# Query features of the later pairs transposed by VectorE and DMA moves instead of TensorE

## The chip, the cores and the metric

The kernel runs on one core of a Trainium2 chip. The metric is the device time of one execution in microseconds; lower is better. TensorE (PE) multiplies, VectorE (DVE), ScalarE (ACT) and GpSimd (POOL) work element by element, SyncE (SP) issues most transfers; ScalarE can issue transfers too.

## The reference

Attention with random features, and behind it two gated feed-forward layers:

```
q, k, v: (4 batches, 8 heads, 576 tokens, 64), omega: (128, 64)
phi(x) = exp(h - max(h)) / sqrt(128),  h = x @ omega.T - |x|^2 / 2   (x scaled)
kv = phi(k).T @ v,  z = sum over tokens of phi(k)
attention = phi(q) @ kv / (phi(q) @ z + 1e-6)
x = attention as (2304 tokens, 512)
h = x @ w_in (512 x 2048);  x = (h * clip(h + 3, 0, 6) / 6) @ w_out (2048 x 512)
h = x @ w_in2;              out = (h * sigmoid(1.702 h)) @ w_out2
```

## The kernel before, in words

Heads are worked on in 16 pairs `a`, four a batch. Pairs 0 to 4 come ahead of the feed-forward layers; pairs 5 to 15 (`a >= LEAD`) are woven into the first layer. Each layer works on five chunks of tokens (four of 512, one of 256) and 16 blocks of 128 inner features (J = 16) a chunk, so step `n` is one block of one chunk: `hidden(n)` makes it (12 matmuls), ScalarE's `gate(n)` and VectorE's `gated_block(n)` gate it, ScalarE's `high(n)` and VectorE's `low(n)` part it in two numbers that add up to it, `output(n)` multiplies it (12 matmuls). Every product is made of three: high by high, low by high, high by low. `hidden(n)` waits for `gated_block(n-1)`, as both use one PSUM bank; `output(n)` waits for `low(n)`. TensorE's order is hidden(n), the units of slot 2n, output(n-1), the units of slot 2n+1.

A pair takes eight slots, `UNITS`. With n0 = 2 + 4(a - 5), slot 0 lies behind output(n0-1), slot 2 (k) behind output(n0), slot 5 (kv) behind hidden(n0+3). The units are: the projections of q with the tails, and of k; the two turns; the key-value sums; two halves of the numerator. After a projection VectorE takes maxima and biases (`statistics`), ScalarE the exponentials (`exps`, tiles of 128 tokens by 128 features). 576 tokens are four tiles and a tail of 64; the tails of two heads share a tile. The numerator needs q's features by feature, not by token: `turn` (L553) transposes four tiles of a head on TensorE, `key_values` (L561) the tail tile; ScalarE copies the turned bank as the high part (L762) and VectorE subtracts it for the low part (L985). `keep` (L972 to L980) parts the sums and the turned tails. The numerator (L614 to L616) makes numerator and denominator at once; `quotient_part` copies them, `normalise` divides.

SP's queue is an order written out by hand: in slot 2 the next pair's key rows, in slot 3 its columns, in slot 6 query rows and values, and in every even slot the weights of step n+5 (until step 15). POOL squares the rows for the norms and makes the weights' low parts, ScalarE the weights' high parts three steps ahead. At the first step of a chunk (`n % J == 0`) both engines evacuate the former chunk's sums; at the last step of a chunk ScalarE (L811) and VectorE (L1063) split the next chunk's input.

Of the kernel before, what the change touches and what calls it, by code (L numbers as in the profile page):

```python
# [11 lines left out]
P = 128  # L12
D = 64
# [9 lines left out]
UNITS = (("q", "tail"), (), ("k",), ("turn0",), ("turn1",), ("kv",), ("nd0",), ("nd1",))  # L23
# [4 lines left out]
def build(nc, q_t, k_t, q_n, k_n, v_n, v_tail, omega_t, w_in, w_out, w_in2, w_out2, out):  # L28
# [24 lines left out]
    with ctx:  # L53
# [32 lines left out]
        q_lo = sb("q_lo", [P, 2, S], F32R)  # L86
# [4 lines left out]
        q_hi = nc.alloc_sbuf_tensor_at("q_hi", [P, 2, S], F32R, offset=(phi_base + 31) // 32 * 32)  # L91
# [32 lines left out]
        turned_out = sem("turned_out")  # L124
        q_lo_ready = sem("q_lo_ready")
# [142 lines left out]
        def tile_of(a, kind, h, t):  # L268

            if t == ST:  # L270
                return (q_tail_b if in_set_b(a) else q_tail_a)[:] if kind == KQ else phi_of(a, kind)[:, 2 * ST * FEAT:GROUPS * FEAT]
            return phi_of(a, kind)[:, (h * ST + t) * FEAT:(h * ST + t + 1) * FEAT]
# [58 lines left out]

        block = ctx.enter_context(nc.Block())

        @block.sync
        def _(sp):
# [40 lines left out]

            sp.dma_start(omega2[0:D, :], omega_t).then_inc(load_omega, 16)
# [121 lines left out]
        def _(pe):  # L499
# [42 lines left out]
            def turn(a, h):  # L542
                pe.wait_ge(exp_done, banks_to(a, "q", h))
                if 0 < a < LEAD - 1 and h == 0:
                    pe.wait_ge(tails_out, a)
                    if a > 1:
                        pe.wait_ge(x_written, 2 * (a - 1))
                elif a < LEAD - 1 and h == 1:
                    pe.wait_ge(turned_out, 2 * a + 1)
                elif a >= LEAD:  # L550
                    pe.wait_ge(exp_done, banks_to(a, "tail", 0) if h == 0 else banks_to(a, "k", 0))
# [4 lines left out]
            def key_values(a):  # L556
# [4 lines left out]
                nc.tensor.transpose(bank[:, 0:P], tile_of(a, KQ, 0, ST), ident[:])  # L561
# [34 lines left out]
            def numerator(a, half):  # L596
                pe.wait_ge(state_ready, a + 1)
                if half == 0:
                    pe.wait_ge(turned_out, 2 * a + 2)
                    if a == LEAD - 1:  # L600
                        pe.wait_ge(gated, 2)
                else:
                    pe.wait_ge(tails_out, a + 1)
                    if a == LEAD - 1:
                        pe.wait_ge(x_written, 2 * a)
# [12 lines left out]
            def attend(a, what):  # L618
                if what in ("q", "k", "tail"):
                    projection(a, what)  # L620
                elif what in ("turn0", "turn1"):
                    turn(a, int(what == "turn1"))
                elif what == "kv":
                    key_values(a)
                else:
# [107 lines left out]
        def _(act):  # L733
# [29 lines left out]

            def first_high(a):
# [16 lines left out]
            def attend(a, what):  # L781
                if what in ("q", "tail", "k"):
                    exps_of(a, what)
                elif what in ("turn0", "turn1"):
                    turned_head(a, int(what == "turn1"))
# [89 lines left out]
            for n in range(2 * L2):  # L875
                former, now = slot_units(2 * n - 1), slot_units(2 * n)
                for a, what in former:
                    if what in ("q", "k"):
                        exps(a, what, 0)
                    elif what != "tail":  # L880
                        attend(a, what)
                gate(n)
                for a, what in former:
                    if what in ("q", "k"):
                        exps(a, what, 1)
                for a, what in now:
# [17 lines left out]
                for a, what in now:  # L904
                    if what not in ("nd0", "nd1"):
# [11 lines left out]
        def _(dve):  # L917
# [40 lines left out]
            def keep(a):  # L958
# [11 lines left out]
                den, num = sums[:, :, D:D + 1].to_broadcast([P, 2, D]), sums[:, :, 0:D]  # L970
                tails, q = bank[:, 0:P].rearrange("p (h s) -> p h s", h=2), q_hi[:, :, ST * P:S]
                nc.vector.tensor_copy(state_hi[:, 1:3, :], den).then_inc(high_set, 1)  # L972
                nc.vector.tensor_copy(state_hi[:, 0:4:3, :], num).then_inc(high_set, 1)
                nc.vector.tensor_copy(q, tails).then_inc(high_set, 1)
                dve.wait_ge(high_set, 3 * (a - LEAD + 1) + 1)
                nc.vector.tensor_tensor(state_lo[:, 1:3, :], den, state_hi[:, 1:3, :].bitcast(F32), ALU.subtract)
                dve.wait_ge(high_set, 3 * (a - LEAD + 1) + 2)
                nc.vector.tensor_tensor(state_lo[:, 0:4:3, :], num, state_hi[:, 0:4:3, :].bitcast(F32), ALU.subtract).then_inc(state_ready, 1)
                dve.wait_ge(high_set, 3 * (a - LEAD + 1) + 3)
                nc.vector.tensor_tensor(q_lo[:, :, ST * P:S], tails, q.bitcast(F32), ALU.subtract).then_inc(tails_out, 1)  # L980
# [67 lines left out]
            def attend(a, what):  # L1048
# [6 lines left out]
                elif what in ("turn0", "turn1"):  # L1055
                    turned_low(a, int(what == "turn1"))
# [80 lines left out]
            for n in range(2 * L2):  # L1137
                before, former, now = (slot_units(2 * n - i) for i in (2, 1, 0))
                for a, what in former:
# [4 lines left out]
                    elif what in ("kv", "turn0", "turn1"):  # L1144
# [4 lines left out]
                gated_block(n)  # L1149
# [5 lines left out]
                for a, what in now:  # L1155
                    if what == "nd0":
                        normalise(a, 0)
                    else:
                        attend(a, what)
                low(n)  # L1160
                if n == 0:
# [65 lines left out]
```

## Time and profile before

| | us |
|---|---|
| median of 3 runs | 930.99 (930.59 to 931.5) |
| the profiled execution, its own time | 932.24 |
| its span, first to last instruction | 930.4 |
| TensorE busy | 923.9 (99%) |
| VectorE busy | 419.3 (45%) |
| ScalarE busy | 378.8 (41%) |
| GpSimd busy | 170.6 (18%) |

Durations of matmuls overlap, since they are pipelined; what one costs is read from the starts. The granted TensorE clock is at full speed in every slice.

### The profile page before, as it was taken

What the parts mean: (1) busy time and instruction counts of PE and PEld (TensorE: products, weight loads), DVE (VectorE), ACT (ScalarE), POOL (GpSimd) and SP (SyncE); (2) the same over time, 40 slices, a digit from 0 to 9 for tenths busy, and PEclk for the clock granted to TensorE, in tenths of its full rate; (3) what the DMA queues carried; (4) which work ended last, traced back from release to release, by engine and by line L of the source; (5) the groups of instructions that cost most, each with busy time, mean ns of one, the idle gap of its engine ahead of it and who ended that gap; (6) DMA issues with size and microseconds to landing.
All of it is one profiled execution on the core that took longest, in us unless ns stands there. A gap on an engine that the chain in (4) does not pass through costs nothing.

```text
span 930.4 us, 13097 instructions
## 1 busy us (share of the span) xinstructions
PE 923.9 (99%) x5130; PEld 785.9 (84%) x5130; DVE 419.3 (45%) x801; ACT 378.8 (41%) x869; POOL 170.6 (18%) x182
## 2 busy tenths in 40 slices
PE   8999999999999999999999999999999999999998
PEld 8988888888888888888889988888888888888898
DVE  6966667655656566532233532242224222422322
ACT  6856565445445454432235732232223222322322
POOL 1765654212122110000007820000000000000000
PEclk9999999999999999999999999999999999999999
DMA  8644341221212210000004600010001000100000
GB/s 273 188 118 132 98 133 27 64 64 39 55 36 64 55 35 14 13 33 1 1 1 137 181 1 1 1 46 1 1 0 46 1 1 0 46 1 1 16 31 24
DMA packets 44254, 46.01 MB, mean 49 GB/s; under 512 B 25120, under 2 KB 25760, under 8 KB 44192
## 3 DMA queue, kind: packets, MB, share of 16 engines
q1 hardware_dynamic: 43680, 44.42, 16.3%
q8 instruction: 41, 0.67, 0.3%
q10 hardware_dynamic: 512, 0.75, 0.3%
q14 instruction: 21, 0.17, 0.1%
HBM read 40.44 MB, written 4.72 MB: 49 GB/s over the span
## 4 chain that ended last, share of the span: by engine, by line
PE 96%; DVE 1%; POOL 1%; DMA 1%; ACT 1%; issue 0%; ACTq 0%; DVEq 0%; POOLq 0%
PE acc L682 14%; PE acc L684 14%; PE acc L683 14%; PE hid L656 11%; PE hid L632 10%; PE hid L657 10%; PE att L657 4%; PE att L656 4%; PE att L632 4%; PE att L569 3%; PE att L531 3%; PE att L553 1%; PE acc L531 1%; PE att L517 1%; PE att L614 1%; PE att L616 1%
## 5 line engine op out<-in xcount | busy, mean ns | idle before, releaser
L682 PE MATMUL acc<-g_hi,w_out_hi 128*128 128x512 f32 (+1 forms) x640 | 237.7, 371 | 0.1
L684 PE MATMUL acc<-g_hi,w_out_lo 128*128 128x512 f32 (+1 forms) x640 | 235.9, 369 | 0.0
L683 PE MATMUL acc<-g_lo,w_out_hi 128*128 128x512 f32 (+1 forms) x640 | 235.6, 368 | 0.0
L656 PE MATMUL hid<-x_hi,w_in_hi 128*128 128x512 f32 (+1 forms) x476 | 179.2, 376 | 0.9 <-DVE R L1071 0.8
L657 PE MATMUL hid<-x_hi,w_in_lo 128*128 128x512 f32 (+1 forms) x476 | 175.2, 368 | 0.0
L632 PE MATMUL hid<-x_lo,w_in_hi 128*128 128x512 f32 (+1 forms) x476 | 175.2, 369 | 0.0
L1078 DVE TENSOR_TENSOR g_lo<-R,g_hi 128x512 fp32r<-128x512 f32 (+1 forms) x160 | 107.9, 674 | 82.8 <-ACT g_hi L828 82.6
L684 PEld LDWEIGHTS acc<-g_hi,w_out_lo 128*128 128x128 f32 x640 | 120.6, 188 | 20.4
L682 PEld LDWEIGHTS acc<-g_hi,w_out_hi 128*128 128x128 f32 x640 | 120.8, 189 | 19.4 <-issue 0.5
L683 PEld LDWEIGHTS acc<-g_lo,w_out_hi 128*128 128x128 f32 x640 | 120.8, 189 | 18.9
L828 ACT ACTIVATE g_hi<-R 128x512 fp32r<-128x512 f32 (+1 forms) x160 | 94.8, 592 | 84.6 <-DVE R L1073 52.6
L656 PEld LDWEIGHTS hid<-x_hi,w_in_hi 128*128 128x128 f32 x476 | 89.7, 189 | 16.4 <-DVE R L1071 1.6
L632 PEld LDWEIGHTS hid<-x_lo,w_in_hi 128*128 128x128 f32 x476 | 89.8, 189 | 15.5 <-DVE x_lo L1038 0.2
L657 PEld LDWEIGHTS hid<-x_hi,w_in_lo 128*128 128x128 f32 x476 | 89.9, 189 | 13.6
L1071 DVE SCALAR_TENSOR_TENSOR R<-R,hid 128x512 f32<-128x512 f32 (+1 forms) x79 | 49.8, 631 | 107.7 <-ACT R L819 107.7
L819 ACT ACTIVATE R<-hid 128x512 f32<-128x512 f32 (+1 forms) x79 | 43.9, 556 | 105.1 <-PE hid L632 105.1
L1073 DVE TENSOR_TENSOR R<-R,hid 128x512 f32<-128x512 f32 (+1 forms) x40 | 25.4, 634 | 112.9 <-ACT R L821 112.9
L1073 DVE TENSOR_TENSOR R<-R,att 128x512 f32<-128x512 f32 (+1 forms) x40 | 25.4, 634 | 112.8 <-ACT R L821 112.8
L821 ACT ACTIVATE R<-att 128x512 f32<-128x512 f32 (+1 forms) x40 | 22.2, 555 | 116.8 <-PE att L632 116.2
L821 ACT ACTIVATE R<-hid 128x512 f32<-128x512 f32 (+1 forms) x40 | 22.2, 555 | 115.9 <-PE hid L632 115.9
L1044 DVE RECIPROCAL k_phi<-k_phi 128x288 f32<-128x288 f32 x24 | 46.8, 1949 | 31.6 <-ACT k_phi L774 31.6
L657 PE MATMUL att<-x_hi,w_in_lo 128*128 128x512 f32 (+1 forms) x164 | 60.4, 368 | 0.0
(165 smaller groups left out, 1096.8 us busy)
## 6 DMA issues: line engine op xcount, KB each, us to landing
X<-w_in SPq DMA_DIRECT2D x16, 256.0 KB, 2.6
X<-w_out SPq DMA_DIRECT2D x16, 256.0 KB, 2.9
out_t<-X SPq DMA_DIRECT2D x16, 256.0 KB, 2.2
rows<-q_n SPq DMA_DIRECT2D x13, 288.0 KB, 3.2
rows<-k_n SPq DMA_DIRECT2D x13, 288.0 KB, 3.0
v_rows<-v_n SPq DMA_DIRECT2D x14, 256.0 KB, 3.3
q_cols<-q_t SPq DMA_DIRECT2D x11, 256.0 KB, 2.5
k_cols<-k_t SPq DMA_DIRECT2D x11, 256.0 KB, 2.7
```

What stands on the lines that cost most here:

```text
L632: return nc.tensor.matmul(hid_bank(n)[:, 0:t], w_hi[0][:, s * 512 + k * P:s * 512 + (k + 1) * P], x_lo[:, k, x0:x0 + t], start=False, stop ...
L656: nc.tensor.matmul(bank, w_hi[0][:, at], x_hi[:, k, x0:x0 + t], start=(k == 0), stop=False)
L657: nc.tensor.matmul(bank, w_lo[0][:, at], x_hi[:, k, x0:x0 + t], start=False, stop=False)
L682: nc.tensor.matmul(bank, w_hi[1][:, at], g_hi[:, g, 0:t], start=(s == 0), stop=False)
L683: nc.tensor.matmul(bank, w_hi[1][:, at], g_lo[:, g, 0:t], start=False, stop=False)
L684: last = nc.tensor.matmul(bank, w_lo[1][:, at], g_hi[:, g, 0:t], start=False, stop=(s == J - 1))
L821: nc.scalar.activation(R[:, 0:t], h, ACT.Sigmoid, scale=1.702).then_inc(gate_ready, 1)
L828: nc.scalar.activation(g_hi[:, n % G_SLOTS, 0:t], R[:, 0:t], ACT.Copy).then_inc(g_hi_ready, 1)
L1044: nc.vector.reciprocal(d, d).then_inc(recip_done, 1)
L1071: nc.vector.scalar_tensor_tensor(out=r, in0=r, scalar=6.0, in1=h, op0=ALU.min, op1=ALU.mult).then_inc(gated, 1)
L1073: nc.vector.tensor_tensor(r, r, h, ALU.mult).then_inc(gated, 1)
L1078: nc.vector.tensor_tensor(g_lo[:, n % G_SLOTS, 0:t], R[:, 0:t], g_hi[:, n % G_SLOTS, 0:t].bitcast(F32), ALU.subtract).then_inc(g_ready, 1)
```

## The change

For pairs 5 to 15 TensorE transposes nothing more. Host code rotates the tokens of the second head by 64 in these pairs (`in_order`), and q's tiles are laid out as head 0, the shared tail, head 1. VectorE transposes the 32x32 blocks of the whole q buffer in two instructions (`cross`, 512 and 640 columns) into `q_blocks`. Then sixteen DMAs (`block_move`), each of 32 partitions by 9 groups by 32 elements, put the blocks in their places in the q buffer: SP issues the twelve off the diagonal, ScalarE the four on it. ScalarE copies each head's 576 columns as the high part (`parts0`, `parts1`), VectorE subtracts for the low part. `keep` no longer handles tails.

The order around it changes too. SP issues the next pair's key rows in slot 1, then waits for `cross` and issues its twelve moves, ahead of the columns and the weights. ScalarE's four moves come at the end of step n0+2, the parts at step n0+3. At the first step of a chunk VectorE's gated product stands ahead of the key statistics, and ScalarE's gate and high part ahead of the key exponentials.

```diff
-UNITS = (("q", "tail"), (), ("k",), ("turn0",), ("turn1",), ("kv",), ("nd0",), ("nd1",))
+UNITS = (("q", "tail"), ("cross",), ("k",), ("moves",), (), ("parts0", "kv", "parts1"), ("nd0",), ("nd1",))
...
-        q_lo = sb("q_lo", [P, 2, S], F32R)
+        blocks_base = nc.sbuf_base
+        q_blocks = sb("q_blocks", [P, 2 * S])
...
+        def block_move(i, j):
+            to = phi_a[KQ][j * 32:(j + 1) * 32, :].rearrange("p (g c) -> p g c", g=GROUPS)
+            blocks = q_blocks[i * 32:(i + 1) * 32, :].rearrange("p (g c) -> p g c", g=GROUPS)
+            return to[:, :, i * 32:(i + 1) * 32], blocks[:, :, j * 32:(j + 1) * 32]
...
+            def moves(a):
+                sp.wait_ge(crossed, 2 * (a - LEAD) + 2)
+                for i in range(4):
+                    for j in range(4):
+                        if j != i:
+                            sp.dma_start(*block_move(i, j)).then_inc(moved[i], 16)
...
             for g in range(2 * LAST1):
-                a = at_slot(g, 2)
+                a = at_slot(g, 1)
                 if a is not None and LEAD <= a < PAIRS - 1:
                     rows_of(a + 1, KK)
+                if a is not None and LEAD <= a:
+                    moves(a)
                 a = at_slot(g, 3)
...
-                nc.tensor.transpose(bank[:, 0:P], tile_of(a, KQ, 0, ST), ident[:])
+                if a < LEAD:
+                    nc.tensor.transpose(bank[:, 0:P], tile_of(a, KQ, 0, ST), ident[:])
...
+            def moves(a):
+                act.wait_ge(crossed, 2 * (a - LEAD) + 2)
+                for i in range(4):
+                    nc.scalar.dma_start(*block_move(i, i)).then_inc(moved[i], 16)
+
+            def high_features(a, h):
+                for i in range(4):
+                    act.wait_ge(moved[i], 64 * (a - LEAD + 1))
+                nc.scalar.activation(q_hi[:, h, :], phi_a[KQ][:, h * S:(h + 1) * S], ACT.Copy).then_inc(turned_out, 1)
...
-                former, now = slot_units(2 * n - 1), slot_units(2 * n)
+                former, now, first = slot_units(2 * n - 1), slot_units(2 * n), n % J == 0
                 for a, what in former:
                     if what in ("q", "k"):
-                        exps(a, what, 0)
+                        if not first:
+                            exps(a, what, 0)
...
                 gate(n)
+                if first:
+                    high(n)
                 for a, what in former:
                     if what in ("q", "k"):
+                        if first:
+                            exps(a, what, 0)
                         exps(a, what, 1)
                 for a, what in now:
-                    if what in ("nd0", "nd1"):
+                    if what in ("nd0", "nd1", "parts0"):
                         attend(a, what)
                 if n % J == J - 1 and n < 2 * L2 - 1:
                     next_chunk(n)
-                high(n)
+                if not first:
+                    high(n)
...
-                if n % J == 0 and n > 0:
+                if first and n > 0:
                     evacuate(n // J - 1)
+                for a, what in now:
+                    if what == "moves":
+                        moves(a)
...
+            def cross(a):
+                split_at = ST * FEAT
+                dve.wait_ge(exp_done, banks_to(a, "q", 0))
+                nc.vector.transpose(q_blocks[:, 0:split_at], phi_a[KQ][:, 0:split_at]).then_inc(crossed, 1)
+                dve.wait_ge(exp_done, banks_to(a, "tail", 0))
+                nc.vector.transpose(q_blocks[:, split_at:2 * S], phi_a[KQ][:, split_at:2 * S]).then_inc(crossed, 1)
+
+            def low_features(a, h):
+                dve.wait_ge(turned_out, 2 * a + h + 1)
+                nc.vector.tensor_tensor(q_lo[:, h, :], phi_a[KQ][:, h * S:(h + 1) * S], q_hi[:, h, :].bitcast(F32),
+                                        ALU.subtract).then_inc(q_lo_ready, 1)
...
+                if n % J == 0:
+                    gated_block(n)
                 for a, what in former:
                     if what in ("q", "k"):
                         attend(a, what)
...
-                gated_block(n)
+                if n % J > 0:
+                    gated_block(n)
...
                 low(n)
+                for a, what in now:
+                    if what == "cross":
+                        attend(a, what)
```

## Rows read from the trace of the kernel before

**Rows 1.** The waits of TensorE, the longest: total us, times, longest.
```profile
PE att L540 <- DVE state L1091: 1.1, 1, 1.1
```

**Rows 2.** Timeline of TensorE, first transposes of pairs 6 and 10.
```profile
105.25 0.60 PE L553 MATMUL att<-ident,q_phi 128*128 128x128 f32 x4
...
224.00 0.60 PE L553 MATMUL att<-ident,q_phi 128*128 128x128 f32 x4
```

**Rows 3.** Instructions of line L553: duration ns min/median/max, first and last start us.
```profile
L553 PE MATMUL att<-ident,q_phi x104: 270/272/328, 9.8 to 375.9; 128*128 128x128 f32 x104
```

**Rows 4.** Timeline of TensorE in pair 10: start us, duration us, instruction.
```profile
223.77 0.39 PE L632 MATMUL hid<-x_lo,w_in_hi 128*128 128x512 f32 x1
...
224.67 0.39 PE L683 MATMUL acc<-g_lo,w_out_hi 128*128 128x512 f32 x1
...
226.97 0.39 PE L684 MATMUL acc<-g_hi,w_out_lo 128*128 128x512 f32 x1
...
227.87 0.39 PE L657 MATMUL hid<-x_hi,w_in_lo 128*128 128x512 f32 x1
...
230.18 0.39 PE L632 MATMUL hid<-x_lo,w_in_hi 128*128 128x512 f32 x1
...
230.74 1.90 PE L569 MATMUL att<-v_rows,k_phi 128*128 128x65 f32 x16
...
235.31 0.29 PE L614 MATMUL att<-q_hi,state_hi 128*128 128x288 f32 x1
```

**Rows 5.** Timeline of VectorE in pair 10.
```profile
219.61 0.69 DVE L1078 TENSOR_TENSOR g_lo<-R,g_hi 128x512 fp32r<-128x512 f32 x1
...
221.25 1.29 DVE L933 TENSOR_REDUCE row_max<-att 128x4 f32<-128x512 f32 x2 [0.74 <-PE att L531]
...
222.85 0.17 DVE L951 SCALAR_TENSOR_TENSOR bias<-h_max,half_norm 128x8 f32<-128x8 f32 x1
224.83 0.69 DVE L1071 SCALAR_TENSOR_TENSOR R<-R,hid 128x512 f32<-128x512 f32 x1 [1.80 <-ACT R L819]
...
232.68 0.29 DVE L972 CAST state_hi<-att 128x128 fp32r<-128x128 f32 x1 [0.75 <-PE att L569]
```

**Rows 6.** The page's groups of instructions: count, busy us, mean ns, idle before.
```profile
L1044 DVE RECIPROCAL k_phi<-k_phi 128x288 f32<-128x288 f32 x24 | 46.8, 1949 | 31.6 <-ACT k_phi L774 31.6
```

**Rows 7.** Timeline of ScalarE in pair 10.
```profile
223.06 1.14 ACT L756 ACTIVATE k_phi<-att,bias 128x128 f32<-128x128 f32 x4 [2.83 <-DVE bias L951]
224.20 0.60 ACT L819 ACTIVATE R<-hid 128x512 f32<-128x512 f32 x1
```

**Rows 8.** Transfers of lines L358, L346 (column tails), L427 (stores): ns, landing us.
```profile
L358 SPq DMA_DIRECT2D rows<-k_n x13: 333/429/1314, 10.4 to 323.9; - x13
...
L346 SPq DMA_DIRECT2D q_cols<-q_t x11: 596/597/597, 48.9 to 340.9; - x11
...
DMA to landing us min/median/max: 2.1/2.2/3.7
...
DMA to landing us min/median/max: 1.7/2.0/2.5
```

**Rows 9.** Windows: stretch, busy us of engines, clock, DMA share, GB/s.
```profile
353.00:354.00 1.00, 1.00 (x6) 0.83 (x5) 0.50 (x2) 0.00 (x0) 0.00 (x0) 1.00 0.99 226
```

**Rows 10.** Timeline of VectorE in pair 6.
```profile
103.90 0.35 DVE L948 SCALAR_TENSOR_TENSOR h_max<-row_max,half_norm 128x8 f32<-128x8 f32 x1
104.29 1.21 DVE L951 SCALAR_TENSOR_TENSOR bias<-h_max,half_norm 128x8 f32<-128x8 f32 x1
```

**Rows 11.** Timeline of GpSimd in pair 6.
```profile
104.19 1.29 POOL L458 TENSOR_TENSOR w_out_lo<-X,w_out_hi 128x512 fp32r<-128x512 f32 x1
109.19 1.15 POOL L447 TENSOR_TENSOR rows<-rows 128x576 f32<-128x576 f32 x1 [3.71 <-DMA rows<-k_n]
```

**Rows 12.** Timeline of TensorE in pair 8, behind hidden(16).
```profile
164.48 0.60 PE L553 MATMUL att<-ident,q_phi 128*128 128x128 f32 x4
```

**Rows 13.** Timeline of VectorE in pair 8, the low part of step 15.
```profile
163.31 0.69 DVE L1078 TENSOR_TENSOR g_lo<-R,g_hi 128x512 fp32r<-128x512 f32 x1
```

**Rows 14.** Timeline of ScalarE in pair 8, the evacuation.
```profile
169.40 1.16 ACT L834 ACTIVATE X<-acc 128x512 f32<-128x512 f32 x2
```

More of the change, by code:

```diff
@@ L124, in build @@
         turned_out = sem("turned_out")
+        crossed = sem("crossed")
+        moved = [sem(f"moved{i}") for i in range(4)]
         q_lo_ready = sem("q_lo_ready")
@@ L268, in tile_of @@
         def tile_of(a, kind, h, t):
+            if kind == KQ and a >= LEAD:
+                g = ST if t == ST else h * (ST + 1) + t
+                return phi_of(a, KQ)[:, g * FEAT:(g + 1) * FEAT]
             if t == ST:
@@ L599, in numerator @@
                     pe.wait_ge(turned_out, 2 * a + 2)
-                    if a == LEAD - 1:
+                if a == LEAD - 1:
+                    if half == 0:
                         pe.wait_ge(gated, 2)
-                else:
-                    pe.wait_ge(tails_out, a + 1)
-                    if a == LEAD - 1:
+                    else:
+                        pe.wait_ge(tails_out, a + 1)
                         pe.wait_ge(x_written, 2 * a)
@@ L783, in attend @@
                     exps_of(a, what)
-                elif what in ("turn0", "turn1"):
-                    turned_head(a, int(what == "turn1"))
+                elif what in ("parts0", "parts1"):
+                    high_features(a, int(what == "parts1"))
                 elif what in ("nd0", "nd1"):
@@ L969, in keep @@
                     return
-                den, num = sums[:, :, D:D + 1].to_broadcast([P, 2, D]), sums[:, :, 0:D]
-                tails, q = bank[:, 0:P].rearrange("p (h s) -> p h s", h=2), q_hi[:, :, ST * P:S]
+                den, num, made = sums[:, :, D:D + 1].to_broadcast([P, 2, D]), sums[:, :, 0:D], highs_to(a - 1)
                 nc.vector.tensor_copy(state_hi[:, 1:3, :], den).then_inc(high_set, 1)
                 nc.vector.tensor_copy(state_hi[:, 0:4:3, :], num).then_inc(high_set, 1)
-                nc.vector.tensor_copy(q, tails).then_inc(high_set, 1)
@@ L980, in keep @@
-                nc.vector.tensor_tensor(q_lo[:, :, ST * P:S], tails, q.bitcast(F32), ALU.subtract).then_inc(tails_out, 1)
+                if a < LEAD:
+                    tails, q = bank[:, 0:P].rearrange("p (h s) -> p h s", h=2), q_hi[:, :, ST * P:S]
+                    nc.vector.tensor_copy(q, tails).then_inc(high_set, 1)
+                    dve.wait_ge(high_set, made + 3)
+                    nc.vector.tensor_tensor(q_lo[:, :, ST * P:S], tails, q.bitcast(F32), ALU.subtract).then_inc(tails_out, 1)
@@ L1054, in attend @@
                         take_tails(a - 1)
-                elif what in ("turn0", "turn1"):
-                    turned_low(a, int(what == "turn1"))
+                elif what == "cross":
+                    cross(a)
+                elif what in ("parts0", "parts1"):
+                    low_features(a, int(what == "parts1"))
             def split(c, blocks_k=range(KC), part=None):
@@ L1143, in _ @@
                         normalise(a, 0)
-                    elif what in ("kv", "turn0", "turn1"):
+                    elif what == "kv":
                         attend(a, what)
@@ L1157, in _ @@
                         normalise(a, 0)
-                    else:
+                    elif what != "cross":
                         attend(a, what)
                 low(n)
+                for a, what in now:
+                    if what == "cross":
+                        attend(a, what)
                 if n == 0:
@@ L1187, with in_order @@
     pairs, full = B * H // 2, S // P
+    def in_order(x):
+        y = x.reshape(pairs, 2, S, Dh).copy()
+        y[LEAD:, 1] = np.roll(y[LEAD:, 1], full * P - S, axis=1)
+        return y
     def cols(x):
-        return np.ascontiguousarray(x.transpose(0, 1, 3, 2).reshape(pairs, 2 * Dh, S))
+        return np.ascontiguousarray(in_order(x).transpose(0, 1, 3, 2).reshape(pairs, 2 * Dh, S))
     def tiles(x):
-        y = x.reshape(pairs, 2, S, Dh)
+        y = in_order(x)
         return y[:, :, :full * P].reshape(pairs, 2, full, P, Dh), y[:, :, full * P:]
```

18 lines of the change are left out of this document (8 added, 10 removed).

## The prediction

> **What bounds the kernel.** In the table above TensorE is busy all through, VectorE and ScalarE less than half. I then read TensorE's waits: none is over 1.1 us [rows 1]. So the end moves by work taken off TensorE or by waits put onto it. The timelines of one pair, at 212 to 240 us (pair 10), show how near each helper is to its due time. Pair 6's first transposes start at 105.25, pair 10's at 224.00: 29.7 us a pair [rows 2]. Every time below is read, or shifted, in such a timeline.
>
> **Taken off TensorE.** L553 transposes eight tiles a pair, L561 one; eleven pairs (5 to 15) lose them, 88 of the first kind among these [rows 3]. Matmuls of 512 columns start 0.23 us apart: ten intervals from 224.67 to 226.97 [rows 4]. Over the first four transposes, from 223.77 to the second matmul behind them at 224.67, it is 0.90 where two starts take 0.46: 0.44 us. Over the second four 0.90 again: 0.44. Over the tail's 0.56 less 0.46: 0.10. Sum 0.98 a pair, times 11 = **10.8 us**, all of it on the engine that bounds. The copies and subtractions that read turned PSUM banks become ones of 576 SBUF columns, about 0.7 us as now.
>
> **Added to VectorE: two 32x32 transposes, 512 and 640 columns, behind the low part of step n0+1.** No row shows this operation. Nearest: the two-input subtraction of 512 columns, 0.69 us, the next start after 0.6; at the near end a maximum, 1.29 for two of 512 [rows 5]; far off the reciprocal, 1.95 for 288 columns, so 7.8 us for 1152 [rows 6]. I take the subtraction's rate, since this too is a plain stream: 0.6 + 0.8 = 1.4 us. Behind them stand the norms (0.2) and the key maxima: 219.61 + 0.6 + 1.4 + 0.2 = 221.8 for 221.25, some 0.6 late. Late next: key exponentials at 223.7 for 223.06, gate at 224.8 [rows 7], gated product ended at 226.1 (now 224.83 + 0.69). Hidden block n0+3 waits for that product and now comes at 226.97 - 0.44 + 0.23 = 226.76. Covered, 0.6 to spare.
>
> **Added to the queues: sixteen moves of 36 KB, 288 pieces of 128 B each.** SP issues twelve once the blocks are ready (221.7). Issues took 0.33 to 1.31 us on SP; the half-width column tails, which the moves resemble most, landed 2.2 after issue, 3.7 at the longest, stores out of SBUF at 1.7 at the least [rows 8]. I take 0.6 with the gap for an issue (between the median 0.43 and the long ones) and 2.3 for landing. SP's last move starts at 221.7 + 11 x 0.6 = 228.3, landed 230.6. The transfer engines' own time: values are 1152 pieces of 256 B a pair, drained around 353 to 355 in some 1.4 us of all sixteen, 0.99 of it in one us [rows 9]; that is 20 ns a piece on one engine. At that price the moves take 288 x 20 ns = 5.8 us of each engine, inside the issue time. ScalarE issues its four after the high part of n0+2: exponentials 223.7, gate 224.8, second half 225.3, high 226.2 to 226.9; last issue 228.7, landed 231.0. Queued behind its issues (2.4 us, to 229.3) is gate(n0+3), whose hidden block ends at 230.18 + 0.23 - 0.88 = 229.5: in time. Behind SP's twelve (7.2 us) wait the next pair's columns, query rows and values: the columns land near 235, and two more blocks of TensorE follow the numerator (235.31) before they are read. Nobody waits.
>
> **The parts.** ScalarE: head 0 from 231.0 to 231.7, high(n0+3) to 232.3, head 1 to 232.9. VectorE: low of head 0 to 232.5, the state's four operations 0.2 apart (as from 232.68, [rows 5]) to 233.3, low of head 1 to 234.0. The numerator's first head is due at 235.31 - 0.98 = 234.3, its second at 234.7 [rows 4]. Covered, by 0.7. So the ordinary pairs (9, 10, 11, 13, 14, 15) keep their 0.98, but a landing more than 0.7 later is paid for one to one.
>
> **Pairs 5 to 7**, where POOL still splits weights. Pair 6's bias, a small operation of two SBUF inputs, took 1.21 us and ended with POOL's subtraction at 105.5; in pair 10 the same is 0.17 [rows 5, 10, 11]. Now the first of the two small operations (103.90) comes 1.35 later, at 105.25, still behind that subtraction, and POOL, whose key rows SP now loads ahead of the moves, goes straight on with a square of 1.15 us, where it had idled until 109.19 [rows 11]. The bias ends at 106.7 for 105.5 and the gated product, by pair 10's steps, at 109.1, while hidden(n0+3) is due 118.8 before pair 10's, at 108.0: 1.1 to 1.2 in pairs 6 and 7, by the same sum 0.85 in pair 5. Together **3.2 us**. The numerator, moved back with it, waits for nothing more. The weights behind SP's moves leave up to 7.2 later; they are asked for five steps ahead and split by ScalarE three ahead, so two steps, 14.8 us, cover that and the landing. The Trainium skill's SBUF — State Buffer, section Who interferes with whom, says that a VectorE instruction with two SBUF inputs waits for a GpSimd instruction that reads SBUF; the long bias agrees. By that rule the new low parts can be held too, and the transposes, with one input, can't.
>
> **Pairs 8 and 12, whose step n0+2 opens a chunk.** The low part of step n0+1 comes at 163.31, behind the next chunk's split, 2.8 later against TensorE than in pair 10 (hidden(16) ended at 164.48) [rows 12, 13]; transposes until 165.3. With the gate first the product is done at 166.2, and hidden(17) is due at 167.3: unhurt. But maxima then start at 166.1, biases end 167.9, eight exponentials 170.1, the evacuation of 1.16 [rows 14] 171.1, and only now come ScalarE's issues, to 173.5, the last landed at 175.2. Head 0 175.8, high 176.4, head 1 177.0, state 177.3, low of head 1 177.9. TensorE: hidden(17) to 170.0, key values to 172.1 (0.1 late), output(16) to 175.0; the numerator's second head, due at 175.35, starts at 177.95. 2.7 us, twice: **5.4 us**.
>
> Gate-first moves nothing in other chunks, where no pair's keys are due.
>
> **Sum.** 10.8 - 3.2 - 5.4 = 2.2 us. The profiled execution took 932.24 with a span of 930.40; these become 930.0 and 928.2. The runs shown have a median of 930.99, 1.25 below that execution: **928.8**. Within 0.2% (1.9 us, about what this kernel's measurement tells from no change) is 929.1 to 932.9.
>
> **Rivals.**
> *All hidden.* The biases slip between two POOL instructions (3.2 back), ScalarE issues in 0.36 and landing is at 1.7, so that pairs 8 and 12 keep 1.1 each: 930.99 - 10.8 + 2.2 = 922.4. For: VectorE, ScalarE and the transfer engines are half idle. Against: the long bias is there in every weight pair.
>
> *Late landing, the other side.* Issues at 0.7 (0.3 at the last of four) and the longest landing, 3.7 (1.4): the last move 1.7 later, so 1.0 in six ordinary pairs (6.0), about 1.0 in each early one (3.0), 1.7 in 8 and 12 (3.4): 928.8 + 12.4 = 941.2. It decides from a landing 0.7 later than mine. In its far form a piece costs 40 ns: the moves drain until 222 + 11.5 + 1.7 = 235.2, 4.2 late, 3.5 a pair: 928.8 + 38 = 967. The Trainium skill's DMA: Bandwidth & Descriptors, Rules for kernel authors, warns of a transpose made by a plain DMA with a rearranged pattern, 19 times slower than the hardware's; here VectorE has turned the blocks and 32 elements lie in a row, so I give the far form 3 in 100.
>
> *Slow transposes.* At 2.8 us, twice mine, the biases come 1.4 later: in ordinary pairs the product ends at 227.5 for 226.8, 0.7 in six (4.2); 1.4 in pairs 5 to 7 (4.2) and in 8 and 12 (2.8): 928.8 + 11.2 = 940.0.
>
> **Chances.** Forecast 0.38 (its own range 926 to 931.5; 0.27 faster, 0.11 same). All hidden 0.22, faster. Late landing 0.17, slow transposes 0.13: 0.26 slower, 0.04 same. Mixtures 0.10: 0.03 faster, 0.03 same, 0.04 slower. Together 0.52 faster, 0.18 same, 0.30 slower. The range is 921 to 942: outside lie full hiding's last us and the far form.
>
> **What the next profile would show.** 99 transposes fewer on TensorE; in ordinary pairs no gap at L614 and a period of 28.7. VectorE's transposes near 0.7 and 0.8, ScalarE's last move landed 9.3 after their end. A gap near 1 us ahead of hidden(n0+3) in pairs 5 to 7, ended by the gated product; gaps of 2.6 at the numerator in pairs 8 and 12, ended by the state or q_lo. If the numerator waits in ordinary pairs, landing was my error; if a hidden block waits there, the transposes; if pairs 8 and 12 don't wait, ScalarE's issues.

## The result and the profile after

The changed kernel takes 934.72 us (median of 7 runs, 933.4 to 935.87) against 931.32 for the kernel before on the same chip: ratio 1.0036, 95% interval 1.0027 to 1.0046. It is slower by 3.4 us; the forecast was 928.8. The profiled execution took 935.54 us with a span of 933.7, so the span (first to last instruction) grew by 3.3. Both profiled executions lie a little above their medians, by 0.8 and 0.9.

The seven runs of the changed kernel fall into two groups: 933.4, 933.72, 933.98 and 934.72 with a mean granted clock of 0.998, and 935.44, 935.54 and 935.87 with 0.996. The runs of the kernel before whose clock is on record show 1.000. Below it turns out that each step of 0.002 is one fall of TensorE's clock; the profiled execution has two.

The page of the changed kernel: totals (busy us, share, instructions) and the chain that ended last.

```profile
PE 918.7 (98%) x5031; PEld 777.7 (83%) x5031; DVE 437.4 (47%) x801; ACT 380.1 (41%) x869; POOL 169.0 (18%) x182
...
PE 82%; DVE 7%; SPq 4%; issue 2%; ACT 2%; DMA 2%; ACTq 0%; POOL 0%; DVEq 0%; POOLq 0%
```

TensorE lost 5.2 us of busy time, yet its part of the chain that ended last fell from 96% to 82%: VectorE and SP's queue now hold parts of it. TensorE's waits (total, times, longest), against [rows 1]:

```profile
PE att L642 <- DVE state_lo L1023: 4.9, 5, 2.0
PE hid L682 <- DVE R L1138: 2.6, 3, 1.0
PE att L642 <- DVE q_lo L1044: 1.7, 2, 1.0
```

L642 is the numerator, L682 the hidden block, L1138 the gated product, L1023 the state's low part, L1044 the new low parts of the features. The new operations, by line (ns minimum, median, maximum), with the landing of the moves:

```profile
L1038 DVE STREAM_TRANSPOSE q_blocks<-q_phi x11: 697/704/705, 72.0 to 374.0; 128x512 f32<-128x512 f32 x11
...
L1040 DVE STREAM_TRANSPOSE q_blocks<-q_phi x11: 795/801/803, 72.7 to 374.7; 128x640 f32<-128x640 f32 x11
...
L402 SPq DMA_DIRECT2D q_phi<-q_blocks x132: 586/614/1997, 73.5 to 382.8; - x132
...
DMA to landing us min/median/max: 1.9/2.0/3.7
...
L1044 DVE TENSOR_TENSOR q_lo<-q_phi,q_hi x22: 741/757/1715, 84.4 to 387.1; 128x576 fp32r<-128x576 f32 x22
```

Transposes, issues and landings are near the values taken. The low parts have a median of 0.76 us and a maximum of 1.7; SP's longest issue took 2.0 us for a median of 0.61.

**Where the time went.** The measure used from here on is the period of a pair: the distance between the starts of two q projections in TensorE's timeline.

| pair | 5 | 6 | 7 | 8 | 9 | 10 | 11 | 12 | 13 | 14 |
|---|---|---|---|---|---|---|---|---|---|---|
| before | 29.61 | 29.61 | 29.62 | 29.90 | 29.62 | 29.61 | 29.61 | 29.90 | 29.61 | 29.61 |
| after | 30.80 | 30.83 | 30.56 | 32.86 | 28.52 | 29.41 | 28.76 | 32.90 | 28.52 | 29.44 |

The ledger below explains the 3.3 us by which the span grew. The undisturbed pairs, 9 and 13, gain 1.09 us (28.52 for 29.61). Eleven of these are 12.0. Pairs 5 to 7 lie 2.28, 2.31 and 2.04 above 28.52: 6.6. Pairs 8 and 12 lie 4.05 and 4.09 above 28.81 (28.52 and the 0.29 which opening a chunk costs before too): 8.1. Pairs 10, 11 and 14 lie 0.89, 0.24 and 0.92 above: 2.05. From pair 15's start to the end the span is 2.17 shorter (567.04 for 569.21): 1.09 is that pair's own gain, and 1.08 goes with a gap of 0.85 at 505.65 in the trace of before that no other trace has there. Pair 5 starts 0.43 earlier. -12.0 + 6.6 + 8.1 + 2.05 - 1.08 - 0.43 = 3.3, the growth of the span.

**Pair 6**, VectorE and POOL, against [rows 10, 11]:

```profile
106.29 1.07 DVE L998 SCALAR_TENSOR_TENSOR bias<-h_max,half_norm 128x8 f32<-128x8 f32 x1
...
114.92 1.58 DVE L1044 TENSOR_TENSOR q_lo<-q_phi,q_hi 128x576 fp32r<-128x576 f32 x1
...
117.22 1.52 DVE L1044 TENSOR_TENSOR q_lo<-q_phi,q_hi 128x576 fp32r<-128x576 f32 x1
```

```profile
106.19 1.15 POOL L476 TENSOR_TENSOR rows<-rows 128x576 f32<-128x576 f32 x1
...
114.59 1.30 POOL L487 TENSOR_TENSOR w_out_lo<-X,w_out_hi 128x512 fp32r<-128x512 f32 x1
116.84 1.29 POOL L487 TENSOR_TENSOR w_in_lo<-X,w_in_hi 128x512 fp32r<-128x512 f32 x1 [0.96 <-ACT w_in_hi L832]
118.09 1.80 POOL L487 TENSOR_TENSOR w_out_lo<-X,w_out_hi 128x512 fp32r<-128x512 f32 x1
```

What TensorE makes of it:

```profile
109.89 0.47 PE L682 MATMUL hid<-x_hi,w_in_hi 128*128 128x512 f32 x1 [1.00 <-DVE R L1138]
...
118.80 0.40 PE L642 MATMUL att<-q_hi,state_hi 128*128 128x288 f32 x1 [0.76 <-DVE q_lo L1044]
```

The bias lies under POOL's square, as forecast, and the hidden block comes late: 1.39 us between starts (108.50 to 109.89) where 0.23 is usual, so 1.16. But both low parts, forecast at 0.7, take 1.6 and 1.5 beside POOL's subtractions of weights, and the numerator's second head starts the moment the second of them ends (117.22 + 1.52).

Set against pair 9 matmul by matmul, the hidden block costs 0.8, 1.2 and 1.3 in pairs 5, 6 and 7 (3.3 together) and the numerator 1.4, 1.1 and 0.8 (3.3 together). The low parts of these pairs last 1.13 and 1.72, 1.58 and 1.52, 1.36 and 0.74.

**Pair 8**, which starts 2.92 later in this trace than in before (156.25 for 153.33). SP's queue, ScalarE's and TensorE's lines:

```profile
168.29 7.88 SPq L402 DMA_DIRECT2D q_phi<-q_blocks  x12
176.21 0.60 SPq L363 DMA_DIRECT2D q_cols<-q_t  x1
```

```profile
170.99 0.59 ACTq L794 DMA_DIRECT2D q_phi<-q_blocks  x1
...
171.76 1.16 ACT L782 ACTIVATE k_phi<-att,bias 128x128 f32<-128x128 f32 x4
...
173.20 0.65 ACTq L794 DMA_DIRECT2D q_phi<-q_blocks  x1
...
177.65 0.68 ACT L799 ACTIVATE q_hi<-q_phi 128x576 fp32r<-128x576 f32 x1 [3.10 <-DMA q_phi<-q_blocks]
```

```profile
177.63 0.39 PE L710 MATMUL acc<-g_hi,w_out_lo 128*128 128x512 f32 x1
179.97 0.40 PE L642 MATMUL att<-q_hi,state_hi 128*128 128x288 f32 x1 [1.96 <-DVE state_lo L1023]
...
181.14 0.40 PE L682 MATMUL hid<-x_hi,w_in_hi 128*128 128x512 f32 x1
...
182.86 0.63 PE L658 MATMUL hid<-x_lo,w_in_hi 128*128 128x512 f32 x1
...
185.49 0.30 PE L642 MATMUL att<-q_hi,state_hi 128*128 128x288 f32 x1
```

ScalarE's last issue ends at 173.85, SP's twelfth at 176.17; the parts start 177.65, so SP's column of twelve issues is the late one. ScalarE's issues run beside the exponentials and the evacuation that stand ahead of them, not behind their ends. The gap of 1.96 is 2.34 between starts (less 0.23: 2.1); with small steps at the matmuls behind it, 2.4 of the pair's 4.05 (see the run fill). Then the next hidden block takes 4.35 us (181.14 to 185.49), where twelve matmuls take 2.7. Its windows (the column behind POOL's is the granted clock, as a share of full speed):

```profile
180.00:182.00 2.00, 2.00 (x9) 1.59 (x10) 1.40 (x3) 1.27 (x4) 0.00 (x0) 0.91 0.63 175
182.00:184.00 2.00, 2.00 (x6) 1.61 (x5) 1.62 (x1) 0.35 (x1) 1.01 (x1) 0.50 1.00 220
184.00:186.00 2.00, 2.00 (x9) 1.61 (x9) 1.17 (x2) 0.31 (x1) 1.75 (x4) 0.74 0.33 116
```

0.50 is the lower level, 1.2 GHz. The same happens behind pair 12's gap of 1.98 (299.55). In this profiled execution both pairs are hit; the four runs at 0.998 have, by that mean, one fall, and on average they are 1.7 us shorter than the three at 0.996 (934.0 for 935.6). The Trainium skill, TensorE: Matmul & The Clock Gate, section HAM oscillation — how this bites in real kernels, says that a wait for data can drop the clock to half; this trace agrees, although the waits of its example are longer than these of 2 us.

### The profile page after: what moved, and what is told of

Its sections match the earlier page's. It is cut to its first block, busy times and chain, and to the rows that moved or that the text cites. A ratio compares the mean times of both kernels' runs of the same rounds, so it can differ in the third digit from the quotient of the medians.

```text
span 933.7 us, 13097 instructions
## 1 busy us (share of the span) xinstructions
PE 918.7 (98%) x5031; PEld 777.7 (83%) x5031; DVE 437.4 (47%) x801; ACT 380.1 (41%) x869; POOL 169.0 (18%) x182
## 4 chain that ended last, share of the span: by engine, by line
PE 82%; DVE 7%; SPq 4%; issue 2%; ACT 2%; DMA 2%; ACTq 0%; POOL 0%; DVEq 0%; POOLq 0%
PE acc L708 12%; PE acc L710 12%; PE acc L709 12%; PE hid L682 9%; PE hid L658 9%; PE hid L683 9%; SPq L402 4%; PE att L682 4%; PE att L658 4%; PE att L683 4%; PE att L560 2%; DMA q_phi<-q_blocks 1%; PE att L597 1%; DVE row_max L980 1%; PE att L642 1%
## 5 line engine op out<-in xcount | busy, mean ns | idle before, releaser
L682 PE MATMUL hid<-x_hi,w_in_hi 128*128 128x512 f32 (+1 forms) x476 | 179.4, 377 | 2.6 <-DVE R L1138 2.6
L1145 DVE TENSOR_TENSOR g_lo<-R,g_hi 128x512 fp32r<-128x512 f32 (+1 forms) x160 | 110.6, 691 | 91.3 <-ACT g_hi L865 91.1
L1138 DVE SCALAR_TENSOR_TENSOR R<-R,hid 128x512 f32<-128x512 f32 (+1 forms) x79 | 49.8, 631 | 121.7 <-ACT R L856 121.7
L682 PEld LDWEIGHTS hid<-x_hi,w_in_hi 128*128 128x128 f32 x476 | 90.7, 190 | 19.2 <-issue 4.0
L682 PE MATMUL att<-x_hi,w_in_hi 128*128 128x512 f32 (+1 forms) x164 | 60.4, 368 | 0.0
```

Of the source, the lines that this page charges most:

```text
L682: nc.tensor.matmul(bank, w_hi[0][:, at], x_hi[:, k, x0:x0 + t], start=(k == 0), stop=False)
L1138: nc.vector.scalar_tensor_tensor(out=r, in0=r, scalar=6.0, in1=h, op0=ALU.min, op1=ALU.mult).then_inc(gated, 1)
L1145: nc.vector.tensor_tensor(g_lo[:, n % G_SLOTS, 0:t], R[:, 0:t], g_hi[:, n % G_SLOTS, 0:t].bitcast(F32), ALU.subtract).then_inc(g_ready, 1)
```

## The experiments

All kernels start from the changed one. Code is shown in cuts. "Gate-first" is the change's new order at a chunk's first step. In the first, second and third below host code reorders the second head's tokens of the crossed pairs along another axis, so that the values differ; the work on the chip is the same.

**Pairs 5 to 7 back on TensorE (t567).** A set TURNED names pairs that keep the old eight slots and TensorE's transposes:

```diff
+OLD_UNITS = (("q", "tail"), (), ("k",), ("turn0",), ("turn1",), ("kv",), ("nd0",), ("nd1",))
+TURNED = (5, 6, 7,)
...
-                    units += [(a, u) for u in UNITS[at]]
+                    units += [(a, u) for u in (UNITS if crossed_pair(a) else OLD_UNITS)[at]]
```

> Pairs 5, 6 and 7 get their transposes on TensorE back, with their old order of units; pairs 8 to 15 keep the new way. Theory: in these three pairs the new way costs more than it saves (periods of 30.8, 30.8 and 30.6 us, where the kernel before had 29.6), because the bias and the two low parts of the features wait for GpSimd's instructions on the weights. Then the periods of pairs 5 to 7 are 29.6 again, and the time is 934.7 - 3.4 = 931.3 us. Rival: what costs is the moves' traffic and SyncE's queue as such, all along; then pairs 5 to 7 gain at most the 1.1 us each that their transposes cost them, and the time stays within 1 us of 934.7.

Measured 931.13 us (930.05 to 933.34), ratio to before 0.9998 [0.999, 1.0007]. Periods of pairs 5 to 7: 29.62, 29.61, 29.61. Crossing them had cost 1.19, 1.22 and 0.94 net, 3.35 together, as much as the whole loss of 3.4: what the other pairs gain and lose cancels. The time is the one expected, and the rival's (within 1 us of 934.7) is out. Its other figure, at most 1.1 us a pair, fits the periods as well, so that the cause has to come from another run (memw).

**Pairs 8 and 12 back on TensorE (t812).** TURNED = (8, 12,).

> Only pairs 8 and 12, whose step n0+2 opens a chunk, get TensorE's transposes back. Theory: their numerators wait some 2.4 us for the parts, and the clock of TensorE then falls to half for some 4 us, which costs 1.6 us more. Periods of 32.9 become 29.9, both: 934.7 - 5.9 = 928.8 us, and the granted clock is 1.000 all through. Rival: the fall of the clock has nothing to do with these gaps; then it shows in this run too, somewhere, and the gain is about 2.7 us: 932.0.

932.43 us (931.42 to 936.21), ratio 1.0012 [1.0004, 1.0021]: a miss by 3.6. The time lies near the rival's 932.0, but the rival itself is out: the granted clock of the profiled execution is 1.000. Periods of 8 and 12 are 31.15 and 30.94, not 29.9, which is 2.3 of the miss; the rest is open. The wait that is new:

```profile
PE att L593 <- ACT k_phi L799: 2.5, 2, 1.3
```

A turned pair's transposes stand behind key exponentials that gate-first has moved back.

**Pairs 5 to 8 and 12 back (t56789).** TURNED = (5, 6, 7, 8, 12,).

> Pairs 5 to 8 and 12 get TensorE's transposes back; 9, 10, 11, 13, 14 and 15 keep the new way. If the losses of both groups are their own, the two gains add up: 934.7 - 3.4 - 5.9 = 925.4 us, faster than both kernels. If they share a cause (queues, traffic, contention), the sum is smaller than the parts: about 928.

928.78 us (928.31 to 931.1), ratio 0.9975 [0.9966, 0.9985]; 31.13 and 30.94 again in pairs 8 and 12. This is 3.4 above the 925.4 of two separate losses and near the 928 of a shared cause; but 2.3 of the 3.4 is again the new wait, not a shared cause, as the next run shows.

**The same without gate-first (best5).** Added to the kernel above:

```diff
-                former, now, first = slot_units(2 * n - 1), slot_units(2 * n), n % J == 0
+                former, now, first = slot_units(2 * n - 1), slot_units(2 * n), False
...
-                if n % J == 0:
-                    gated_block(n)
...
-                if n % J > 0:
-                    gated_block(n)
+                gated_block(n)
```

> Pairs 5 to 8 and 12 by TensorE's transposes, as in t56789, and the gate no longer first at a chunk's first step. Theory: in t56789 the periods of pairs 8 and 12 are 31.1 and 30.9 us, since the second turn waits for the key exponentials that now stand behind the gate (1.34 and 1.15 us). In the old order they are 29.9: 928.8 - 2.3 = 926.5 us, below both kernels. Rival: the old order costs something elsewhere in pair 8 or 12 with the other parts of the change in; then 928 to 929.

925.94 us (925.56 to 926.67), ratio 0.9945 [0.9933, 0.9958]: faster than both kernels, as expected (926.5). Pairs 8 and 12 are at 29.89 and 29.90, as before. Pairs 9 and 13 still lose 0.5 and 0.85; in these SP's twelve issues took 8.82 and 9.19 us, where 7.9 is usual.

**Gate-first undone in the changed kernel (keysfirst).** The same edit, all pairs crossed.

> The changed kernel with the gate behind the first key exponentials at a chunk's first step too, as in the kernel before. Theory: in pairs 8 and 12 two things are late by the same 2.4 us, the gated product (key biases at 170.1, first exponentials 171.2, gate 171.8, product 172.5 against a hidden block due at 170.1) and the last move (landed 177.6), and the second is late against a numerator that the first moves back; one wait takes the place of the other: 934.7, within 0.7, with the gap now ahead of the hidden block. Rival: the gate's place is worth its wait, and the two add: 934.7 + 4.8 = 939.5.

935.36 us (934.33 to 936.11), ratio 1.0044 [1.0031, 1.0057]. Pairs 8 and 12: 32.91 and 32.69. The wait only moves, from the numerator to the hidden block, as expected:

```profile
174.23 0.79 PE L682 MATMUL hid<-x_hi,w_in_hi 128*128 128x512 f32 x1 [2.63 <-DVE R L1138]
```

**The gap filled (fill).** Nine multiplications of the identity by itself (18 in the trace) stand ahead of the numerator in pairs 8 and 12; nothing reads them.

```diff
+            FILL = {8: 9, 12: 9}
...
+                if half == 0:
+                    for _ in range(FILL.get(a, 0)):
+                        nc.tensor.matmul(head_bank(a, 0, 0)[:, 0:P], ident[:], ident[:], start=True, stop=True)
```

> The changed kernel with nine matmuls of 128 columns (float32, results overwritten) ahead of the numerator in pairs 8 and 12, where TensorE stands idle for 2.1 us; nine should take 1.9 us. Theory: TensorE's gap is what lets the clock fall, so with the gap filled the granted clock stays at 1.000, the hidden block behind the numerator takes 2.7 us instead of 4.3, and the time is 934.7 - 3.2 = 931.5 us. Rival: the clock falls for another reason (the moves, the transposes missing); then the fall is still there and the time is 934.7 or, if the filling overruns the gap, a few tenths more.

932.35 us (931.26 to 937.63), ratio 1.0018 [1.0006, 1.003]. The filler runs from 177.46, the numerator follows without a gap, and the window that had 0.50 has full clock (2.4 GHz):

```profile
177.46 2.17 PE L629 MATMUL att<-ident 128*128 128x128 f32 x18
179.57 0.40 PE L647 MATMUL att<-q_hi,state_hi 128*128 128x288 f32 x1
```

```profile
182.00:184.00 2.00, 2.00 (x13) 1.72 (x11) 1.97 (x2) 0.34 (x1) 1.28 (x2) 1.00 0.88 179
```

Periods 31.24 and 31.26: 1.62 and 1.64 less, with the numerator just as late. That is the clock's share in a pair that it hits; 2.4 of the 4.05 is the wait's. The medians give only 2.4 of these 3.3 back: four of the seven runs of the changed kernel had one fall and not two, and three of the twelve here still show 0.998 (935.39 to 937.63).

**POOL's subtractions of weights replaced by a fill with zeros (memw).** The low parts of the first layer's weights are left out; the fill reads nothing.

```diff
-                nc.gpsimd.tensor_tensor(w_lo[kind][:, at], raw, w_hi[kind][:, at].bitcast(F32),
-                                        ALU.subtract).then_inc(w_ready, 1)
+                nc.gpsimd.memset(w_lo[kind][:, at].bitcast(F32), 0.0).then_inc(w_ready, 1)
```

> The changed kernel with zeros written by GpSimd in place of the low parts of all weights (a memset reads nothing; the waits stay). The low parts of the weights are left out of the result. Theory: in pairs 5 to 7 VectorE's two low parts of the features last 1.5 us in place of 0.75 because GpSimd's subtraction of the weights reads SBUF at that time; with the memset they last 0.75, the numerator's second head waits no more (0.8 to 1.0 us now), and the periods of pairs 5 to 7 fall from 30.8 to 29.8 or less, some 3 us in all: 931.7. Rival: the long low parts have another cause (the moves' traffic into the same buffer), nothing changes in pairs 5 to 7: 934.7.

929.2 us (927.55 to 932.34), ratio 0.9979 [0.9968, 0.999], 2.5 below what was expected. Periods of 5 to 7: 28.60, 28.52, 28.91. In pair 6 VectorE now has

```profile
103.40 0.52 DVE L997 SCALAR_TENSOR_TENSOR bias<-h_max,half_norm 128x8 f32<-128x8 f32 x1
...
112.08 0.76 DVE L1043 TENSOR_TENSOR q_lo<-q_phi,q_hi 128x576 fp32r<-128x576 f32 x1 [0.75 <-ACT q_hi L798]
...
113.55 0.74 DVE L1043 TENSOR_TENSOR q_lo<-q_phi,q_hi 128x576 fp32r<-128x576 f32 x1
```

So nearly the whole loss of pairs 5 to 7 (6.6 in the changed kernel, 0.5 now) comes with POOL's two-input work on the weights: the low parts are short again, the second (113.55) even beside a write of zeros by POOL (0.53 us from 113.73), so that it is the reads that held it. And since writing zeros takes 0.53 for 1.29, POOL's square of the rows ends ahead of the bias (at 103.13 in pair 6). The weights still leave behind SP's moves; of the 0.5, 0.39 is pair 7's, whose twelve issues took 8.70. The rule of the Trainium skill that the prediction weighed (SBUF — State Buffer, Who interferes with whom) agrees with this: the low parts have two SBUF inputs, and the prediction's own sentence that they "can be held too" was the one to put a price on.

**SP's column shortened (split6).** ScalarE takes two more moves, (3,0) and (3,1), at the place where it issued four.

```diff
+ACT_MOVES = [(0, 0), (1, 1), (2, 2), (3, 3), (3, 0), (3, 1)]
...
-                        if j != i:
+                        if (i, j) not in ACT_MOVES:
...
-                for i in range(4):
-                    nc.scalar.dma_start(*block_move(i, i)).then_inc(moved[i], 16)
+                for i, j in ACT_MOVES:
+                    nc.scalar.dma_start(*block_move(i, j)).then_inc(moved[i], 16)
```

SP keeps ten of the sixteen.

> ScalarE issues six of the sixteen moves, SyncE ten. Theory: the moves are late by SyncE's issues, 0.66 us each and one after another, and not by the engines that carry them; SyncE's last move lands 1.3 us sooner. In pairs 8 and 12 the parts start at 176.6 for 177.6: 1.0 us less each; in ordinary pairs ScalarE's last move is then the late one, about where SyncE's was: no change. 934.7 - 2.0 = 932.7. Rival: the transfer engines are the limit (288 pieces an engine); then nothing lands sooner and the time stays at 934.7.

951.59 us (947.76 to 953.22), ratio 1.0213 [1.0194, 1.0232]: far off. Where the theory was made for, it holds: in pairs 8 and 12 the parts start 0.9 sooner after the pair's start, the gap is 1.05 for 1.96, the clock doesn't fall, and the periods are 30.36 and 30.37 for 32.86 and 32.90. All other crossed pairs ahead of the last lose: pairs 5 to 7 take 34.3, 34.4 and 34.7, pair 14 33.35. In pair 9 SP is through with its moves and starts columns of 256 KB while ScalarE still issues:

```profile
212.14 3.32 ACTq L795 DMA_DIRECT2D q_phi<-q_blocks  x5
...
213.85 0.61 SPq L364 DMA_DIRECT2D q_cols<-q_t  x1
...
218.43 0.69 ACT L800 ACTIVATE q_hi<-q_phi 128x576 fp32r<-128x576 f32 x1 [2.27 <-DMA q_phi<-q_blocks]
```

ScalarE's issues end at 215.46 (212.14 + 3.32), so the sixth begins near 214.8, and the parts start 3.6 later. The longest landing on its queue is 4.7 us. In pairs 5 to 7 and 14 the gap at the numerator is 2.5 to 2.7 us, and the clock falls behind each of the four, at some 1.6 apiece: about 6 of the loss against the kernel before is the clock's. The next run asks whether the loads make the landings late.

**SP holds its loads until the moves have landed (split6hold).** Added to the kernel above, behind SP's moves:

```diff
+                for i in range(4):
+                    sp.wait_ge(moved[i], 64 * (a - LEAD + 1))
```

> The run before it, with SyncE's last two moves given to ScalarE (six each), took 951.6 us, and ScalarE's last moves landed 3.5 us after their issue where 2.1 was usual. Here the same split, but SyncE waits until all twelve moves have landed before it issues its loads of columns and weights. Theory A, the 256 KB loads that start earlier share the DMA queues with the last small moves and hold them up: the landing goes back to near 2.1 us, and the time to 934 us or below (the changed kernel's 934.7). Theory B, ScalarE's own longer column of issues (its share of the moves, and its exponentials behind them) is what costs: the landing may be short but the time stays at about 948 to 952 us.

936.12 us (933.51 to 936.96), ratio 1.0054 [1.0037, 1.007]. Fifteen us are back, by one wait; ScalarE's share of the moves is the same (six, with ten on SP; the expectation's "six each" is a slip), so it wasn't that. Part of the fifteen is the clock: the four falls are gone from the profiled execution, and the other three runs (0.998) have one by their mean clock. The median is 1.4 above the changed kernel's and not below, though the intervals overlap, and the longest landing is still 4.0. Pairs 5 to 7 take 31.4 to 31.8, 0.6 to 1.3 more than in the changed kernel. There ScalarE's column has become the late one: in pair 5 its six issues end at 83.63 and the last lands at 85.03, SP's ten have landed by 82.86, and the parts start 11.3 after SP's first issue for 10.1. Whether the weights, which leave later still, add to it wasn't tried. Pairs 8 and 12 are at 30.29 and 30.34 with a gap of 1.0 at the numerator and no fall of the clock. The section Rules for kernel authors of the Trainium skill's DMA: Bandwidth & Descriptors says that transfers spread over SP and ScalarE interleave on the same 16 engines and save issue time only; in split6 that saving shows in pairs 8 and 12 and is lost elsewhere to the loads that it let start sooner.

**ScalarE's moves one step earlier, alone (actearly).**

```diff
-                    if what == "moves":
+                    if what == "cross":
```

> ScalarE's four moves are issued one step earlier, at the end of the step that holds the transposes, as its block stood before. Theory A: SyncE's twelfth move is the one that lands last, so nothing is gained, and the key exponentials behind the four issues start later by up to 4 x 0.6 us less their slack: between no change and 2 us slower than the changed kernel, 934.7 to 937. Theory B: ScalarE's moves are the late ones: the pairs with a late numerator get about 0.9 us back in pairs 10 and 14 and up to 2.4 in pairs 8 and 12, 928 to 932 us.

936.13 us (934.97 to 936.88), ratio 1.005 [1.0035, 1.0065]: theory A. In pair 10, which starts 0.15 earlier here, the parts start at 237.19 (237.17 in the changed kernel), although ScalarE's four issues begin at 226.32 and not at 230.72: SP's moves set the landing. SP's twelve even take a little longer beside them, 8.2 us in pairs 9, 12, 13 and 15 where 7.9 was usual. The waits have changed places, with the numerator down from 4.9 to 0.7 and the hidden block up from 2.6:

```profile
PE hid L682 <- DVE R L1138: 10.6, 7, 2.1
...
PE att L642 <- DVE state_lo L1023: 0.7, 2, 0.4
```

**SP's moves behind the slot's weights (spafter).** The two lines of `moves(a)` in SP's loop stand behind the weight loads.

> SyncE's twelve moves stand after the slot's weight loads in place of before them. Theory A: the moves start later by three issues of 0.6 us in the pairs with weights, 5 to 7 (1.8 us each, and in those pairs the heads' second numerator is held by VectorE's low parts already, so that some of it is hidden): 935 to 940 us. Theory B: the last landing is hidden in these pairs behind the low parts, and the weights landing earlier let the low parts start earlier: no change, 934 to 935 us, or a gain of up to 1 us.

935.88 us (934.31 to 937.64), ratio 1.0049 [1.0034, 1.0064]. Pairs 5 to 7 take 31.07, 31.18, 31.28: 0.27, 0.35 and 0.72 more, 1.3 in all. In pair 6 the moves start at 107.31, 11.79 after the pair's start, against 9.55 in the changed kernel. Of a start 2.2 later only 0.35 is paid, since one wait takes another's place: the low parts (117.56 and 119.03) now come when POOL rests, last 0.76 and 0.74, and the numerator waits for the landing. The time lies at the low end of theory A; the interval still overlaps with no change.

## Why the prediction was wrong

**Right.** The mechanism of the saving: 1.09 a pair, forecast 0.98; blocks behind transposes had been dearer by 0.1. The transposes: 0.70 and 0.80 us, spaced 0.63 and 0.72, against 0.6 + 0.8, with no hidden block late in ordinary pairs. Twelve issues take 7.88, 0.66 each (taken: 0.6), landing 2.0 (taken: 2.3). The transfer engines stay inside the issue time. The bias of pairs 5 to 7 lies behind POOL and costs 1.2 at the hidden block in pairs 6 and 7, as forecast (3.3 in three pairs for 3.2). Gate-first leaves hidden(17) unhurt.

**The step that failed** is the one for pairs 5 to 7, "The numerator, moved back with it, waits for nothing more". The low parts were priced at 0.7 in every pair. Here five of the six take 1.1 to 1.7, two in a row ahead of the numerator in pairs 5 and 6, one in pair 7: the numerator costs 3.3 more in three pairs where nothing was put (6.6 in all for 3.2). The paragraph named the rule by which they could be held and left the sum as it was; POOL's subtractions stood in the trace of before, beside pair 6's numerator (116.56):

```profile
114.04 1.30 POOL L458 TENSOR_TENSOR w_out_lo<-X,w_out_hi 128x512 fp32r<-128x512 f32 x1
115.29 1.75 POOL L458 TENSOR_TENSOR w_in_lo<-X,w_in_hi 128x512 fp32r<-128x512 f32 x1
117.00 1.29 POOL L458 TENSOR_TENSOR w_out_lo<-X,w_out_hi 128x512 fp32r<-128x512 f32 x1
```

[rows 5, 10] gave the price of one such meeting, about 1.0 (1.21 for 0.17). By that estimate two meetings, less the slack of 0.7, are 1.4 in each of three pairs: 4.2 for the 3.4 that was missing. memw shows the cause, t567 the size.

**Mis-sized: pairs 8 and 12**, 5.4 for 8.1. The wait at the numerator was 2.4 for 2.7, but not by the step given. The parts waited for SP's twelve issues (7.88 us), which the prediction had landing a microsecond ahead of ScalarE's; ScalarE's issues didn't stand behind its evacuation. Two errors, a late SP and an early ScalarE, nearly cancelled. What the sum lacked is the clock: 1.6 each where it falls, shown by fill; both pairs in the profiled execution (3.3), one of them in four of the seven runs. A wait of 2 us was priced at 2 us.

**Mis-sized: the ordinary pairs**, 0 for 2.05. From SP's first issue to the start of the parts 9.3 us was forecast, and 9.36 to 9.57 it is in pairs 8, 9, 12, 13 and 15 (7.88 of issues and 1.48 in pair 8). But in pairs 10, 11 and 14 it is 10.70, 9.95 and 10.75: the twelve issues take up to 9.3, or, as in pair 10, the column's issue right behind them takes 1.72 for 0.60 and the parts start 2.53 after the twelfth. The maximum of an issue is 2.0 us for a median of 0.61. The cover was put at 0.7 against a steady column; it had to hold one long issue too, 0.5 to 1.4 longer than the others. In size this is a third of what the rival of late landing put on the six ordinary pairs (6.0).

What makes an issue long wasn't tried, but the traces point at one thing. The twelve-issue column of pair 14 holds the longest one (2.0 us at 351.35), and in that stretch, 350 to 353, the DMA queues show a transfer of the program's own instructions (16 KB, queue q8):

```profile
q8 instruction: 1, 0.02, 3.1%
```

In all thirteen traces together SP makes 3153 issues between 60 and 400 us. 152 of them overlap such a transfer in time, and all 43 that last over 1.2 us are among these. So issues as long as that came only with such a transfer; many beside one stayed short, and that it is the cause is not shown.

**Not in the sum:** 1.1 us gained late in the span by a gap that vanished (505.65), in every one of the other kernels. Why it was there is open; it may belong to that one execution, which lies 0.9 above the median of its kernel. Another 0.4 was gained ahead of pair 5.

By the forecast's own terms: the saving was 12.0 for 10.8 and the other two gains gave 1.5, but the losses were 16.8 (6.6 + 8.1 + 2.05) for 8.6.

## What to carry to other kernels

Moving work off the bounding engine is worth its whole time only where the detour fits: here it gained 1.09 us in some pairs and lost 1 to 3 in others, and the version that chose pair by pair and kept the old order of the gate (925.94) beat both. Price each two-input VectorE operation beside GpSimd's reads at about twice its length (0.75 us became 1.1 to 1.7 here), and count how many lie between a late input and its reader. Where a wait of two microseconds on TensorE is forecast, reckon with the clock's fall too (1.6 us here). Check what a queue starts once its small moves are done.

## What was not expected of the hardware

A gap's length alone does not tell whether the clock falls: behind 1.96 us (pair 8 of the changed kernel) it fell, behind 2.03 (pair 8 of t567, period 31.35) it didn't, behind 2.33 (pair 12 of t567, period 33.26) it did again. In actearly two gaps of the same 2.11 us, at the hidden blocks of pairs 8 and 12, had it fall behind the first and not behind the second. ScalarE's DMA issues run beside the activations that stand ahead of them in its program: the one at 173.20 overlaps the evacuation's second half; the gate behind them starts only at 173.95, with the last issue done. Small moves between SBUF buffers, landed in 2.0 us as a rule (median), took up to 4.7 with 256 KB loads started beside them from another queue, and the kernel 15.5 us more, about 5 of it through the clock; one wait took that away.
